# Masks moved into spare contraction rows of an attention kernel's score products

## The chip, the cores and the metric

The kernel runs on one core of one Trainium2 chip. The metric is the device time of the whole program in microseconds; of several executions the median is given. The core has five engines with an instruction queue each: TensorE (PE; its weight loads are listed apart, as PEld), VectorE (DVE), ScalarE (ACT), GpSimd (POOL) and SyncE (SP), which here only issues transfers.

## The reference

Attention comes first, then a product of two linear layers, then a layer of eight experts of which each token takes two. The change touches only attention. There are 4 batches of 8 heads, 576 positions and 64 values a head.

```
scores = (q @ k.T) / sqrt(64)
scores = where(pos_q // 64 >= pos_k // 64, scores, -1e9)
attn = exp(scores - max(scores)); attn = attn / (sum(attn) + 1e-9)
out = attn @ v
x = concat of the heads, 2304 x 512
x = ((x @ w1) * (x @ w2) @ w3) @ w_out
out = sum over the two best experts e of weight * (relu(x @ e_w1[e]) @ e_w2[e])
```

A block of 64 query positions sees its own block of keys and the ones before it.

## The kernel before, in words

Every float32 product is made of rounded parts ("high", in the type fp32r) and what rounding left ("low"), so that three or four products of parts stand for one. The 32 heads go in 16 pairs; `hp` counts the four pairs of a batch, `n` all of them, and `u` is the parity of a pair's buffers. The first batch is written out, the other three are one hardware loop (`batches`). A head's 576 query rows are five tiles of 128, 128, 128, 128 and 64 rows, and tile `i` takes the keys up to its own end: 128, 256, 384, 512 and 576 (the last in two halves of 288). So a pair has ten steps `t`, five for each of its heads.

At each step TensorE makes the scores of tile `t` (`product`), transposes the probabilities of the tile three steps earlier (`turn`), and makes a part of the previous pair's product with v (`values`, in the order of `values_at`). VectorE takes a tile's maximum (L295), and the low part of transposed probabilities (`low`, L250, four steps behind); ScalarE takes the exponentials (L366) and the high part (`high`, L333, three steps behind).

The inputs of the next pair are made ready beside this. SyncE loads q and k, each twice: the 64 values of a head lie on partitions 0 to 63 and again on 64 to 127, both heads side by side, 1152 columns in all. For pair n+1, while pair n is computed:

- GpSimd scales q (L208), once it has cut v of the pair before.
- VectorE rounds q into `q_split` (`q_part`, L273, at step 1) and k into `k_high` (`k_part`, L277, at step 3).
- GpSimd writes what rounding left of q over the upper 64 partitions of `q_split` (L213), and then what is left of k into `k_low` (L217).
- GpSimd then cuts v into its parts (`cut_v`, L226 and L229, two of each).

Since `q_split` holds q's high part on its lower and the low part on its upper 64 contraction rows, and `k_high` holds k twice, one multiplication gives (q_high + q_low) k_high and a second one (q_high + q_low) k_low. Between them stands a third, for tiles 0 to 3: `mask_rows` times `mask_keys`, 64 columns wide, with one contraction row that is not zero, which adds -1e9 to the upper right quarter of the tile's last 128 columns (L399). The fifth tile of keys has 64 positions, and `values` multiplies it over 64 contraction rows (`K = rows[c]`).

At the start, VectorE alone prepares pair 0, once all of its q and k have landed (L307 to L313). The two engines' waits are counted in `q_scaled`, `q_high_ready`, `k_high_ready`, `q_cut` and `k_cut`.

After attention (from about 260 us) come the weights' fusion, the gated product with the routing, and the experts; all of their work starts behind a barrier at attention's end.

Of the kernel before, what the change touches and what calls it, by code (L numbers as in the profile page):

```python
# [5 lines left out]
F32 = mybir.dt.float32  # L6
F32R = mybir.dt.float32r
# [8 lines left out]
def attention(nc, qT, kT, v, identity, xT, prefetch, prefetched):  # L16
# [14 lines left out]
    MASKED = -1e9  # L31
    SCALE = D ** -0.5
    BANKS = 4
# [25 lines left out]
    with ExitStack() as ctx:  # L59
# [9 lines left out]
        q_split = [sb(f"q_split{u}", [P, 2, S], F32R) for u in range(2)]  # L69
        k_high = [sb(f"k_high{u}", [P, 2, S], F32R) for u in range(2)]  # L70
        k_low = [sb(f"k_low{u}", [P, 2, S], F32R) for u in range(2)]
# [6 lines left out]
        mask_rows = sb("mask_rows", [P, P], F32R)  # L78
        mask_keys = sb("mask_keys", [P, BLOCK], F32R)
        mask_raw = sb("mask_raw", [P, P + BLOCK])  # L80
# [16 lines left out]
        waited_pe = sem("waited_pe")  # L97
        qk_loaded = [sem(f"qk_loaded{u}") for u in range(2)]
# [10 lines left out]
        mask_filled = sem("mask_filled")  # L109
        masks_ready = sem("masks_ready")  # L110
        max_found = sem("max_found")
# [9 lines left out]
        out_taken = sem("out_taken")  # L121
        block = ctx.enter_context(nc.Block())
# [14 lines left out]
        def beside(i):  # L137

            return turned[i % TURNED][:, (i + 1) * P:]

# [7 lines left out]
        def _(sp):  # L148
# [11 lines left out]
            for u in range(2):  # L160
                load(u, u)
            sp.dma_start(ident[:], identity).then_inc(ident_loaded, 16)

            def emit(b, first):
                for hp in range(PAIRS):
                    n = b * PAIRS + hp
                    sp.wait_ge(q_cut, n + 1)
                    sp.wait_ge(k_cut, n + 1)

                    load(n + 2, hp % 2)  # L170
                    if first and hp == 0:
                        sp.wait_ge(zeroed, 1)
                    else:
                        sp.wait_ge(v_cut, 2 * n)
# [7 lines left out]
        def _(pool):  # L182
            nc.gpsimd.memset(v_raw[:], 0.0).then_inc(zeroed, 1)
            nc.gpsimd.memset(mask_raw[:], 0.0).then_inc(mask_filled, 1)
            pool.wait_ge(mask_filled, 1)
            nc.gpsimd.memset(mask_raw[0:1, 0:BLOCK], 1.0).then_inc(mask_filled, 1)
            nc.gpsimd.memset(mask_raw[0:1, P:P + BLOCK], MASKED).then_inc(mask_filled, 1)
            nc.gpsimd.memset(scale[:], SCALE).then_inc(zeroed, 1)
            nc.gpsimd.memset(zero[:], 0.0).then_inc(zeroed, 1)
            for u in range(2):  # L190
                nc.gpsimd.memset(row_sum[u][:], 1.0).then_inc(zeroed, 1)
            nc.gpsimd.memset(probs[:], 0.0).then_inc(zeroed, 1)
# [45 lines left out]
            with pool.Fori(1, LAST // 2) as m:  # L238
                for u in range(2):
                    cut_qk(2 * m + u + 1, m + u, 1 - u)  # L240
                    cut_v(2 * m + u, u, False)

        @block.vector
        def _(dve):
# [26 lines left out]
            def q_part(n, u):  # L271
                dve.wait_ge(q_scaled, n + 1)
# [1345 lines left out]
```

## Time and profile before

| | |
|---|---|
| median of three runs | 1150.83 us (1149.87 to 1151.39) |
| the profiled execution: its time | 1149.4 us |
| its span, first to last instruction | 1147.5 us |
| mean granted clock of TensorE | 0.977 |
| busy: PE, PEld, DVE, ACT, POOL | 1078.7, 975.5, 473.9, 371.3, 541.9 us |
| DMA in all | 118.11 MB |

"Busy" is the time in which an engine carries out instructions; a multiplication's end is modelled by the profile, so the start times of neighbours say more of its pace than its duration. In a list in order of time, a row gives start and duration in microseconds, engine, line, operation, the tiles written and read with their shapes (partitions x elements), and in brackets how long the engine had been idle and what it waited for. For a multiplication, 64*128 stands for 64 contraction rows and 128 columns of weights.

### The profile page before, as it was taken

The page shows a single profiled execution, that of the slowest core. Times are in us where ns is not written, and L with a number is a line of the kernel's source. Part 1 is how long each engine was busy: PE and PEld are TensorE (multiplying, and loading weights), DVE is VectorE, ACT ScalarE, POOL GpSimd, SP SyncE. Part 2 cuts the span into 40 slices and gives each one's busy share as a digit, 9 for nine tenths or more (in the row PEclk, how much of TensorE's full clock was granted, in tenths as well). Part 3 has the DMA queues.
Part 4 walks back from the last instruction along what each step waited for, and adds up shares of the span by engine and source line. Part 5 has one row for each costly group of instructions (what it writes and reads, how often), then busy time and mean ns, then how long its engine had stood idle before and what let it go on. Part 6 is the DMA issues. An engine that isn't in the chain of part 4 may idle for free. (4 is left out here: it accounts for less than half of the span.)

```text
span 1147.5 us, 18575 instructions
## 1 busy us (share of the span) xinstructions
PE 1078.7 (94%) x6320; PEld 975.5 (85%) x6321; DVE 473.9 (41%) x1073; ACT 371.3 (32%) x898; POOL 541.9 (47%) x368
## 2 busy tenths in 40 slices
PE   4999999998999999999999549999999999999997
PEld 3888888887798989899999449898989898989895
DVE  5887877866512424241414442222222222222221
ACT  3777777765411213231313142121212121212110
POOL 7776777740000020201111133786878787877752
PEclk9999999998999999999999759999999999999999
DMA  8644444426397010101000063535353535353303
GB/s 230 149 100 92 94 93 101 103 52 195 91 368 278 2 55 0 55 9 46 21 35 34 30 231 128 114 97 144 100 143 117 121 115 123 110 128 119 46 1 46
DMA packets 69638, 118.11 MB, mean 103 GB/s; under 512 B 7776, under 2 KB 25312, under 8 KB 69600
## 3 DMA queue, kind: packets, MB, share of 16 engines
q1 hardware_dynamic: 60960, 97.61, 28.8%
q0 software_dynamic: 8640, 20.00, 8.8%
q8 instruction: 22, 0.36, 0.1%
q14 instruction: 16, 0.13, 0.0%
HBM read 81.00 MB, written 36.59 MB: 102 GB/s over the span
## 5 line engine op out<-in xcount | busy, mean ns | idle before, releaser
L782 POOL DMA_INDIRECT expert_rows<-x_rows,slot_idx x36 | 40.1, 1113 | 311.9 <-DVE slot_idx L925 302.8
L1387 PE MATMUL ps_hT<-xT_high,ew_high 128*128 128x256 f32 (+3 forms) x512 | 156.8, 306 | 1.9 <-DVE xT_low L1473 1.9
L1387 PE MATMUL ps_hT<-xT_low,ew_high 128*128 128x256 f32 (+3 forms) x512 | 155.7, 304 | 0.0
L1387 PE MATMUL ps_hT<-xT_high,ew_low 128*128 128x256 f32 (+3 forms) x512 | 155.2, 303 | 0.0
L1404 PE MATMUL ps_y<-ew_high,hT_high 128*128 128x512 f32 x320 | 129.3, 404 | 1.4 <-DVE hT_low L1480 1.4
L1404 PE MATMUL ps_y<-ew_low,hT_high 128*128 128x512 f32 x320 | 126.9, 397 | 0.0
L1404 PE MATMUL ps_y<-ew_high,hT_low 128*128 128x512 f32 x320 | 126.9, 396 | 0.0
L1480 DVE SCALAR_TENSOR_TENSOR hT_low<-ps_hT,hT_high 128x384 fp32r<-128x384 f32 (+1 forms) x128 | 62.9, 492 | 152.2 <-ACT hT_high L1442 152.2
L1442 ACT ACTIVATE hT_high<-ps_hT 128x384 fp32r<-128x384 f32 (+1 forms) x128 | 56.0, 438 | 156.7 <-PE ps_hT L1387 156.2
L1277 POOL DMA_INDIRECT out<-y_tile,out_rows x40 | 63.1, 1577 | 90.1 <-DVE y_tile L1489 85.8
L1489 DVE TENSOR_SCALAR y_tile<-ps_y,weight_of 128x512 f32<-128x512 f32 x40 | 30.0, 751 | 179.0 <-PE ps_y L1404 179.0
L366 ACT ACTIVATE probs<-scores,neg_max 128x128 f32<-128x128 f32 (+4 forms) x160 | 91.7, 573 | 32.7 <-DVE neg_max L295 32.1
L1387 PEld LDWEIGHTS ps_hT<-xT_high,ew_high 128*128 128x128 f32 x512 | 97.1, 190 | 2.3 <-DVE xT_low L1473 2.3
L1387 PEld LDWEIGHTS ps_hT<-xT_high,ew_low 128*128 128x128 f32 x512 | 97.9, 191 | 0.0
L1387 PEld LDWEIGHTS ps_hT<-xT_low,ew_high 128*128 128x128 f32 x512 | 97.1, 190 | 0.0
L250 DVE TENSOR_TENSOR pT_low<-turned,pT_high 128x128 fp32r<-128x128 f32 (+4 forms) x160 | 76.9, 481 | 29.7 <-ACT pT_high L333 29.7
L1436 ACT CAST xT_high<-ps_xT 128x512 fp32r<-128x512 f32 x40 | 23.5, 587 | 196.4 <-PE ps_xT L1370 196.4
L295 DVE TENSOR_REDUCE neg_max<-scores 128x1 f32<-128x128 f32 (+4 forms) x160 | 85.4, 534 | 3.6 <-PE scores L400 2.4
L932 DVE TENSOR_TENSOR prod<-ps_b,prod 128x384 f32<-128x384 f32 x48 | 26.8, 558 | 130.5 <-ACT prod L811 130.5
L333 ACT CAST pT_high<-turned 128x128 fp32r<-128x128 f32 (+4 forms) x160 | 67.5, 422 | 39.8 <-PE turned L413 35.6
L396 PE MATMUL scores<-k_high,q_split 128*128 128x128 f32 (+2 forms) x192 | 65.7, 347 | 14.1 <-DMA ident_a<-const_in 14.1
L413 PE MATMUL turned<-ident_a,probs 128*128 128x128 f32 (+1 forms) x480 | 73.9, 262 | 4.2 <-DVE pT_low L250 3.2
(198 smaller groups left out, 2683.4 us busy)
## 6 DMA issues: line engine op xcount, KB each, us to landing
spare<-e_w SPq DMA_DIRECT2D x16, 1024.0 KB, 5.3
w_raw<-e_w SPq DMA_DIRECT2D x16, 1024.0 KB, 8.3
q_raw<-qT SPq DMA_DIRECT2D x36, 288.0 KB, 4.3
k_raw<-kT SPq DMA_DIRECT2D x36, 288.0 KB, 5.5
expert_rows<-zeros SPq DMA_DIRECT2D x8, 1290.0 KB, 14.3
ex_rows<-expert_rows SPq DMA_DIRECT2D x40, 258.0 KB, 3.9
out<-zeros SPq DMA_DIRECT2D x11, 512.0 KB, 10.8
v_raw<-v SPq DMA_DIRECT2D x16, 256.0 KB, 4.9
```

Source lines behind the costliest of these rows:

```text
L250: nc.vector.tensor_tensor(pT_low[j][:, 0:i + 1, i * P:i * P + R], turned[t % TURNED][:, 0:(i + 1) * R].rearrange("p (c r) -> p c r", r=R), ...
L295: nc.vector.tensor_reduce(neg_max[0:rows[i], t:t + 1], tile_scores(t), AX.XY if width[i] > 512 else AX.X, ALU.max, negate=True).then_inc(m ...
L333: nc.scalar.copy(pT_high[j][:, 0:i + 1, i * P:i * P + R], turned[t % TURNED][:, 0:(i + 1) * R].rearrange("p (c r) -> p c r", r=R)).then_in ...
L366: nc.scalar.activation(like_scores(probs[0:R, slot, 0:W], t), tile_scores(t), ACT.Exp, bias=neg_max[0:R, t:t + 1], accum_out=row_sum[hp % ...
L396: nc.tensor.matmul(out, lhsT, k_high[u][:, j, a:a + step], start=True, stop=False)
L413: mm = nc.tensor.transpose(turned[t % TURNED][:, c * R:(c + 1) * R], probs[0:R, slot, c * P:(c + 1) * P], ident[0:R, 0:R])
L782: nc.gpsimd.indirect_dma_start(out=rows_dram, out_offset=bass.IndirectOffsetOnAxis(ap=slot_idx[:, k, t:t + 1], axis=0), in_=x_rows[:, t, : ...
L1277: nc.gpsimd.indirect_dma_start(out=out, out_offset=bass.IndirectOffsetOnAxis(ap=out_rows[:, j:j + 1], axis=0), in_=y_tile[j][:], in_offset ...
L1387: mm = nc.tensor.matmul(ps_hT[q % HS][:, 0:rows.stop - rows.start], lhsT[:, c, f * P:(f + 1) * P], rhs[:, c, rows], start=(n == 0), stop=( ...
L1404: mm = nc.tensor.matmul(ps_y[j % YS][:], lhsT[:, f, rows], rhs[:, f], start=(n == 0), stop=(n == 3 * FC - 1))
L1442: nc.scalar.activation(hT_high[:, f, rows], ps_hT[q % HS][:, 0:rows.stop - rows.start], ACT.Relu).then_inc(hhigh, 1)
L1480: nc.vector.scalar_tensor_tensor(out=hT_low[:, f, rows], in0=ps_hT[q % HS][:, 0:rows.stop - rows.start], scalar=0.0, in1=hT_high[:, f, row ...
```

## The change

1. **Masks.** `q_split`, `k_high` and `k_low` are replaced by four tiles. `q_high` holds q's high part on both halves of the partitions. `q_rest` holds q's low part on partitions 0 to 63, and on 64 to 67 four mask rows, loaded from the host once (zeros above). `k_parts` holds k's high part on 0 to 63 and its low part on 64 to 127. `k_again` holds k's high part on 0 to 63 and four mask rows on 64 to 67. So q_high times k_parts gives q_high k_high + q_high k_low, and q_rest times k_again gives q_low k_high and the mask. The masking multiplication is gone, and so is the product of the two low parts.
2. **The copy.** k's high part must stand in `k_again` too. GpSimd issues a DMA from `k_parts` (64 partitions of 4608 bytes) for each pair from 1 on, between its two subtractions; TensorE waits for it (`k_copied`) at step 0. GpSimd's subtraction for k now covers 64 partitions and not 128.
3. **The order of the casts.** k is rounded at step 1 and q at step 2; before, it was q at step 1 and k at step 3.
4. **The fifth key tile** is multiplied over all 128 contraction rows (the upper ones are zero).
5. **The first pair** is loaded head by head, q by SyncE and k by ScalarE's queue, and split head by head by ScalarE and VectorE together. ScalarE also copies the masks into place (four copies of 4 partitions x 1152), after GpSimd has cleared the four tiles.

The diff, cut to its core:

```diff
-        q_split = [sb(f"q_split{u}", [P, 2, S], F32R) for u in range(2)]
-        k_high = [sb(f"k_high{u}", [P, 2, S], F32R) for u in range(2)]
-        k_low = [sb(f"k_low{u}", [P, 2, S], F32R) for u in range(2)]
+        q_high = [sb(f"q_high{u}", [P, 2, S], F32R) for u in range(2)]
+        q_rest = [sb(f"q_rest{u}", [P, 2, S], F32R) for u in range(2)]
+        k_parts = [sb(f"k_parts{u}", [P, 2, S], F32R) for u in range(2)]
+        k_again = [sb(f"k_again{u}", [P, 2, S], F32R) for u in range(2)]
...
-        mask_rows = sb("mask_rows", [P, P], F32R)
-        mask_keys = sb("mask_keys", [P, BLOCK], F32R)
-        mask_raw = sb("mask_raw", [P, P + BLOCK])
...
+        mask_raw = [xT[D:D + MASKS, side, 0:2 * S].rearrange("p (h s) -> p h s", h=2) for side in range(2)]
...
+        def load_first(engine, dst, src, h):
+
+            for half in range(2):
+                engine.dma_start(dst[half * D:(half + 1) * D, h], src[0, h]).then_inc(first_loaded[h], 16)
...
-            for u in range(2):
-                load(u, u)
-            sp.dma_start(ident[:], identity).then_inc(ident_loaded, 16)
+            for side in range(2):
+                sp.dma_start(mask_raw[side], masks[side]).then_inc(masks_loaded, 16)
+            for h in range(2):
+                load_first(sp, q_raw[0], qT, h)
+                if h == 0:
+                    sp.dma_start(ident[:], identity).then_inc(ident_loaded, 16)
+            load(1, 1)
...
-                    sp.wait_ge(q_cut, n + 1)
-                    sp.wait_ge(k_cut, n + 1)
+                    if first and hp == 0:
+                        sp.wait_ge(first_cut, 4)
+                        sp.wait_ge(first_k_again, 2)
+                    else:
+                        sp.wait_ge(q_cut, n)
+                        sp.wait_ge(k_cut, n)
...
-                        sp.wait_ge(zeroed, 1)
+                        sp.wait_ge(zeroed, 4)
...
         def _(pool):
+            nc.gpsimd.memset(q_rest[0][:].bitcast(F32), 0.0).then_inc(masks_zeroed, 1)
+            nc.gpsimd.memset(k_again[0][:].bitcast(F32), 0.0).then_inc(masks_zeroed, 1)
+            nc.gpsimd.memset(q_rest[1][:].bitcast(F32), 0.0).then_inc(masks_zeroed, 1)
+            nc.gpsimd.memset(k_again[1][:].bitcast(F32), 0.0).then_inc(masks_zeroed, 1)
+            nc.gpsimd.memset(probs[:, PSLOTS - 1, S:TILES * P], 0.0).then_inc(zeroed, 1)
+            for u in range(2):
+                nc.gpsimd.memset(row_sum[u][:], 1.0).then_inc(zeroed, 1)
             nc.gpsimd.memset(v_raw[:], 0.0).then_inc(zeroed, 1)
-            nc.gpsimd.memset(mask_raw[:], 0.0).then_inc(mask_filled, 1)
-            pool.wait_ge(mask_filled, 1)
-            nc.gpsimd.memset(mask_raw[0:1, 0:BLOCK], 1.0).then_inc(mask_filled, 1)
-            nc.gpsimd.memset(mask_raw[0:1, P:P + BLOCK], MASKED).then_inc(mask_filled, 1)
             nc.gpsimd.memset(scale[:], SCALE).then_inc(zeroed, 1)
             nc.gpsimd.memset(zero[:], 0.0).then_inc(zeroed, 1)
-            for u in range(2):
-                nc.gpsimd.memset(row_sum[u][:], 1.0).then_inc(zeroed, 1)
-            nc.gpsimd.memset(probs[:], 0.0).then_inc(zeroed, 1)
             for u in range(2):
                 nc.gpsimd.memset(v_high[u][:].bitcast(F32), 0.0).then_inc(zeroed, 1)
             for u in range(2):
                 nc.gpsimd.memset(v_low[u][:].bitcast(F32), 0.0).then_inc(zeroed, 1)
 
...
-                pool.wait_ge(qk_loaded[u], 64 * (half + 1))
+                pool.wait_ge(qk_loaded[u], 64 * (half + u))
                 if first:
-                    pool.wait_ge(zeroed, 9)
-                    pool.wait_ge(q_high_ready, 1)
+                    pool.wait_ge(zeroed, 10)
+                    pool.wait_ge(masks_zeroed, 4)
...
-                if first:
-                    pool.wait_ge(k_cut, 1)
-                    pool.wait_ge(q_cut, 1)
-                pool.wait_ge(q_high_ready, n + 1)
-                nc.gpsimd.tensor_tensor(q_split[u][D:2 * D], q_raw[u][D:2 * D], q_split[u][D:2 * D].bitcast(F32),
-                                        ALU.subtract).then_inc(q_cut, 1)
-                pool.wait_ge(k_high_ready, n + 1)
-                pool.wait_ge(q_cut, n + 1)
-                nc.gpsimd.tensor_tensor(k_low[u][:], k_raw[u][:], k_high[u][:].bitcast(F32), ALU.subtract).then_inc(k_cut, 1)
+                pool.wait_ge(q_high_ready, n)
+                nc.gpsimd.tensor_tensor(q_rest[u][0:D], q_raw[u][0:D], q_high[u][0:D].bitcast(F32), ALU.subtract).then_inc(q_cut, 1)
+                pool.wait_ge(k_high_ready, n)
+                pool.sem_inc(waited_pool, 1)
+                nc.gpsimd.dma_start(k_again[u][0:D], k_parts[u][0:D]).then_inc(k_copied, 16)
+                nc.gpsimd.tensor_tensor(k_parts[u][D:2 * D], k_raw[u][D:2 * D], k_parts[u][D:2 * D].bitcast(F32),
+                                        ALU.subtract).then_inc(k_cut, 1)
...
-                pool.wait_ge(k_cut, n + 2)
...
+            pool.wait_ge(k_copied, 16 * LAST)
...
-                dve.wait_ge(q_scaled, n + 1)
-                nc.vector.tensor_copy(q_split[u][:], q_raw[u][:]).then_inc(q_high_ready, 1)
+                dve.wait_ge(q_scaled, n)
+                nc.vector.tensor_copy(q_high[u][:], q_raw[u][:]).then_inc(q_high_ready, 1)
...
-                dve.wait_ge(qk_loaded[u], 64 * (half + 1))
-                nc.vector.tensor_copy(k_high[u][:], k_raw[u][:]).then_inc(k_high_ready, 1)
+                dve.wait_ge(qk_loaded[u], 64 * (half + u))
+                nc.vector.tensor_copy(k_parts[u][:], k_raw[u][:]).then_inc(k_high_ready, 1)
...
                         if t == 1:
+                            k_part(b * (PAIRS // 2) + (hp + 1) // 2, (hp + 1) % 2)
+                        if t == 2:
                             q_part(n + 1, (hp + 1) % 2)
-                        if t == 3:
-                            k_part(b * (PAIRS // 2) + (hp + 1) // 2, (hp + 1) % 2)
-
-
-            dve.wait_ge(qk_loaded[0], 64)
-            nc.vector.tensor_scalar(q_raw[0][:], q_raw[0][:], SCALE, None, ALU.mult).then_inc(q_scaled, 1)
-            k_part(0, 0)
-            q_part(0, 0)
-            dve.wait_ge(k_high_ready, 1)
-            nc.vector.tensor_tensor(k_low[0][:], k_raw[0][:], k_high[0][:].bitcast(F32), ALU.subtract).then_inc(k_cut, 1)
-            dve.wait_ge(q_high_ready, 1)
-            nc.vector.tensor_tensor(q_split[0][D:2 * D], q_raw[0][D:2 * D], q_split[0][D:2 * D].bitcast(F32),
-                                    ALU.subtract).then_inc(q_cut, 1)
+
+
+            dve.wait_ge(masks_zeroed, 1)
+            for h in range(2):
+                dve.wait_ge(first_loaded[h], 64)
+                nc.vector.tensor_scalar(q_high[0][:, h], q_raw[0][:, h], SCALE, None, ALU.mult).then_inc(first_q_high, 1)
+                dve.wait_ge(first_k_high, h + 1)
+                nc.vector.tensor_tensor(k_parts[0][D:2 * D, h], k_raw[0][D:2 * D, h], k_parts[0][D:2 * D, h].bitcast(F32), ALU.subtract)\
+                    .then_inc(first_cut, 1)
+                dve.wait_ge(first_q_high, h + 1)
+                nc.vector.scalar_tensor_tensor(out=q_rest[0][0:D, h], in0=q_raw[0][0:D, h], scalar=SCALE,
+                                               in1=q_high[0][0:D, h].bitcast(F32), op0=ALU.mult, op1=ALU.subtract).then_inc(first_cut, 1)
...
+                            act.wait_ge(zeroed, 3)
...
-            act.wait_ge(mask_filled, 3)
-            nc.scalar.copy(mask_rows[:], mask_raw[:, 0:P]).then_inc(masks_ready, 1)
-            nc.scalar.copy(mask_keys[:], mask_raw[:, P:P + BLOCK]).then_inc(masks_ready, 1)
+            load_first(act, k_raw[0], kT, 0)
+            load_first(act, k_raw[0], kT, 1)
+            act.wait_ge(masks_loaded, 32)
+            for u in range(2):
+                act.wait_ge(masks_zeroed, 2 * u + 2)
+                nc.scalar.copy(q_rest[u][D:D + MASKS], mask_raw[0]).then_inc(masks_ready, 1)
+                nc.scalar.copy(k_again[u][D:D + MASKS], mask_raw[1]).then_inc(masks_ready, 1)
+            for h in range(2):
+                act.wait_ge(first_loaded[h], 64)
+                nc.scalar.copy(k_parts[0][:, h], k_raw[0][:, h]).then_inc(first_k_high, 1)
+                nc.scalar.copy(k_again[0][0:D, h], k_raw[0][0:D, h]).then_inc(first_k_again, 1)
...
-                if t == 0:
-                    pe.wait_ge(k_cut, n + 1)
-                    pe.wait_ge(q_cut, n + 1)
+                if fresh and i == 0:
+                    pe.wait_ge(first_cut, 2 * j + 2)
+                    pe.wait_ge(first_k_again, j + 1)
+                elif t == 0:
+                    pe.wait_ge(k_cut, n)
+                    pe.wait_ge(q_cut, n)
+                    pe.wait_ge(k_copied, 16 * n)
...
-                lhsT = q_split[u][:, j, i * P:i * P + R]
+                rows_of = slice(i * P, i * P + R)
                 step = HALF if W > 512 else W
                 for a in range(0, W, step):
                     out = scores[0:R, bank[t] + a // step, 0:step]
-                    nc.tensor.matmul(out, lhsT, k_high[u][:, j, a:a + step], start=True, stop=False)
-                    if i < FULL:
-
-                        nc.tensor.matmul(scores[0:R, bank[t], W - BLOCK:W], mask_rows[:], mask_keys[:], start=False, stop=False)
-                    mm = nc.tensor.matmul(out, lhsT, k_low[u][:, j, a:a + step], start=False, stop=True)
+                    nc.tensor.matmul(out, q_high[u][:, j, rows_of], k_parts[u][:, j, a:a + step], start=True, stop=False)
+                    mm = nc.tensor.matmul(out, q_rest[u][:, j, rows_of], k_again[u][:, j, a:a + step], start=False, stop=True)
...
-                K = rows[c]
...
-                    lhsT, rhs = vs[u][0:K, c, j], ps[j][0:K, c]
+                    lhsT, rhs = vs[u][:, c, j], ps[j][:, c]
...
-            pe.wait_ge(masks_ready, 2)
+            pe.wait_ge(masks_ready, 4)
...
+    block = 64
+    place = np.arange(S)
+    masks = np.zeros((2, S // (2 * block), 2, S), np.float32)
+    for i in range(S // (2 * block)):
+        masks[0, i, :, place // block == 2 * i] = 1
+        masks[1, i, :, place // block == 2 * i + 1] = -1e9
```

## Rows read from the trace of the kernel before

**Rows 1.** The page: busy time in tenths of 40 equal slices, TensorE's row.
```profile
PE   4999999998999999999999549999999999999997
```
**Rows 2.** Busy time by engine in a stretch of attention (instructions in brackets), granted clock, DMA share, GB/s.
```profile
180.00:210.00 30.00, 29.89 (x209) 26.74 (x208) 24.04 (x54) 21.91 (x67) 21.42 (x15) 1.00 0.45 98
```
**Rows 3.** Waits from 60 to 240 us: total, times, longest.
```profile
POOL q_split L213 <- DVE q_split L273: 40.7, 13, 3.6
```
**Rows 4.** GpSimd in order of time, one pair: start, duration, instruction, wait before it.
```profile
104.60 2.64 POOL L213 TENSOR_TENSOR q_split<-q_raw,q_split 64x1152 fp32r<-64x1152 f32 x1 [3.59 <-DVE q_split L273]
107.94 2.65 POOL L217 TENSOR_TENSOR k_low<-k_raw,k_high 128x1152 fp32r<-128x1152 f32 x1 [0.70 <-DVE k_high L277]
110.81 0.72 POOL L226 TENSOR_TENSOR v_high<-v_raw,zero_a 128x320 fp32r<-128x320 f32 x1 [0.23 <-POOL k_low L217]
112.56 0.72 POOL L226 TENSOR_TENSOR v_high<-v_raw,zero_a 128x320 fp32r<-128x320 f32 x1
114.29 2.11 POOL L208 TENSOR_TENSOR q_raw<-q_raw,scale 128x1152 f32<-128x1152 f32 x1
119.54 2.65 POOL L213 TENSOR_TENSOR q_split<-q_raw,q_split 64x1152 fp32r<-64x1152 f32 x1 [3.14 <-DVE q_split L273]
```
**Rows 5.** VectorE in order of time, around both casts of the same pair.
```profile
103.77 0.75 DVE L273 CAST q_split<-q_raw 128x1152 fp32r<-128x1152 f32 x1
104.43 0.69 DVE L250 TENSOR_TENSOR pT_low<-turned,pT_high 128x512 fp32r<-128x512 f32 x1
105.03 0.55 DVE L295 TENSOR_REDUCE neg_max<-scores 128x1 f32<-128x384 f32 x1
105.50 0.48 DVE L250 TENSOR_TENSOR pT_low<-turned,pT_high 128x320 fp32r<-128x320 f32 x1
106.77 1.09 DVE L277 CAST k_high<-k_raw 128x1152 fp32r<-128x1152 f32 x1
107.78 0.28 DVE L250 TENSOR_TENSOR pT_low<-turned,pT_high 128x128 fp32r<-128x128 f32 x1
```
**Rows 6.** TensorE's multiplications in order of time, same pair.
```profile
106.49 0.27 PE L447 MATMUL heads_out<-pT_high,v_low 128*128 128x192 f32 x1
106.61 0.27 PE L447 MATMUL heads_out<-pT_low,v_high 128*128 128x192 f32 x1
106.81 0.29 PE L447 MATMUL heads_out<-pT_high,v_high 64*128 64x64 f32 x1
...
110.15 0.28 PE L396 MATMUL scores<-k_high,q_split 128*128 128x256 f32 x1
110.27 0.19 PE L399 MATMUL scores<-mask_keys,mask_rows 128*128 128x64 f32 x1
...
110.49 0.60 PE L413 MATMUL turned<-ident_a,probs 128*128 128x128 f32 x4
...
115.40 0.30 PE L396 MATMUL scores<-k_high,q_split 128*128 128x128 f32 x1
```
**Rows 7.** GpSimd in order of time, in the expert stage.
```profile
714.93 4.61 POOL L1239 TENSOR_TENSOR ew_low<-spare,ew_high 128x2048 fp32r<-128x2048 f32 x1
719.71 1.69 POOL L1277 DMA_INDIRECT out<-y_tile,out_rows  x1 [0.16 <-issue]
720.87 4.16 POOL L1233 TENSOR_TENSOR ew_high<-spare,consts 128x2048 fp32r<-128x2048 f32 x1
...
752.40 3.60 POOL L1233 TENSOR_TENSOR ew_high<-w_raw,consts 128x2048 fp32r<-128x2048 f32 x1
```
**Rows 8.** Instructions of one tensor (ns: min/median/max), and its DMAs' time to landing.
```profile
L782 POOL DMA_INDIRECT expert_rows<-x_rows,slot_idx x36: 963/969/2225, 403.3 to 663.4; - x36
...
DMA to landing us min/median/max: 2.6/3.0/17.1
```
**Rows 9.** All engines in order of time, at the start.
```profile
13.96 2.10 POOL L208 TENSOR_TENSOR q_raw<-q_raw,scale 128x1152 f32<-128x1152 f32 x1 [4.90 <-DMA k_raw<-kT]
14.11 0.48 PE L396 MATMUL scores<-k_high,q_split 128*128 128x128 f32 x1 [14.11 <-DMA ident_a<-const_in]
...
17.18 2.64 POOL L213 TENSOR_TENSOR q_split<-q_raw,q_split 64x1152 fp32r<-64x1152 f32 x1 [1.12 <-DVE q_split L273]
...
18.32 2.12 DVE L277 CAST k_high<-k_raw 128x1152 fp32r<-128x1152 f32 x1
```
**Rows 10.** VectorE in order of time, in the last pair.
```profile
239.55 0.48 DVE L250 TENSOR_TENSOR pT_low<-turned,pT_high 128x320 fp32r<-128x320 f32 x1
```

More of the change, by code:

```diff
@@ L13, with attention @@
 META = 4
-def attention(nc, qT, kT, v, identity, xT, prefetch, prefetched):
+def attention(nc, qT, kT, v, identity, masks, xT, prefetch, prefetched):
     _, _, D, S = qT.shape
@@ L30, in attention @@
     HALF = S // 2
-    MASKED = -1e9
     SCALE = D ** -0.5
+    MASKS = masks.shape[1]
     BANKS = 4
@@ L97, in attention @@
         waited_pe = sem("waited_pe")
+        waited_pool = sem("waited_pool")
         qk_loaded = [sem(f"qk_loaded{u}") for u in range(2)]
@@ L108, in attention @@
         scores_ready = sem("scores_ready")
-        mask_filled = sem("mask_filled")
+        masks_loaded = sem("masks_loaded")
+        masks_zeroed = sem("masks_zeroed")
         masks_ready = sem("masks_ready")
+        first_loaded = [sem(f"first_loaded{h}") for h in range(2)]
+        first_k_high = sem("first_k_high")
+        first_k_again = sem("first_k_again")
+        first_q_high = sem("first_q_high")
+        first_cut = sem("first_cut")
+        k_copied = sem("k_copied")
         max_found = sem("max_found")
@@ L208, in cut_qk @@
                 nc.gpsimd.tensor_tensor(flat, flat, scale[:].to_broadcast([P, 2 * S]), ALU.mult).then_inc(q_scaled, 1)
-                if first:
-                    pool.wait_ge(k_cut, 1)
-                    pool.wait_ge(q_cut, 1)
-                pool.wait_ge(q_high_ready, n + 1)
-                nc.gpsimd.tensor_tensor(q_split[u][D:2 * D], q_raw[u][D:2 * D], q_split[u][D:2 * D].bitcast(F32),
-                                        ALU.subtract).then_inc(q_cut, 1)
-                pool.wait_ge(k_high_ready, n + 1)
-                pool.wait_ge(q_cut, n + 1)
-                nc.gpsimd.tensor_tensor(k_low[u][:], k_raw[u][:], k_high[u][:].bitcast(F32), ALU.subtract).then_inc(k_cut, 1)
+                pool.wait_ge(q_high_ready, n)
[5 more added lines that the diff above has]
+                                        ALU.subtract).then_inc(k_cut, 1)
             def cut_v(n, u, first):
                 pool.wait_ge(v_loaded, 32 * (n + 1))
-                pool.wait_ge(k_cut, n + 2)
+                pool.wait_ge(k_cut, n + 1)
                 if not first:
@@ L364, in emit @@
                         elif t == 0:
-                            act.wait_ge(zeroed, 6)
+                            act.wait_ge(zeroed, 3)
                         nc.scalar.activation(like_scores(probs[0:R, slot, 0:W], t), tile_scores(t), ACT.Exp,
                                              bias=neg_max[0:R, t:t + 1], accum_out=row_sum[hp % 2][0:R, t:t + 1]).then_inc(exp_done, 1)
-            act.wait_ge(mask_filled, 3)
-            nc.scalar.copy(mask_rows[:], mask_raw[:, 0:P]).then_inc(masks_ready, 1)
-            nc.scalar.copy(mask_keys[:], mask_raw[:, P:P + BLOCK]).then_inc(masks_ready, 1)
+            load_first(act, k_raw[0], kT, 0)
[9 more added lines that the diff above has]
+                nc.scalar.copy(k_again[0][0:D, h], k_raw[0][0:D, h]).then_inc(first_k_again, 1)
             batches(act, emit)
@@ L1505, in _, with bass_attention_moe @@
             through(dve, stretch)
-def bass_attention_moe(nc, qT, kT, v, w1, w2, w3T, w_out, w_gate_noise, noise, e_w1, e_w2, const_in, C, out):
+def bass_attention_moe(nc, qT, kT, v, w1, w2, w3T, w_out, w_gate_noise, noise, e_w1, e_w2, const_in, masks, C, out):
     P = 128
@@ L1547, in bass_attention_moe @@
                          (consts[:], const_in), (counts[:], const_in[:, C["start"]:C["start"] + E])]
-            attention(nc, qT, kT, v, const_in[:, C["ident"]:C["ident"] + P], xT, prefetch, prefetched)
+            attention(nc, qT, kT, v, const_in[:, C["ident"]:C["ident"] + P], masks, xT, prefetch, prefetched)
             w1_high, w1_low, w2_high, w2_low = (part(moe, name, DC, F) for name in ("w1_high", "w1_low", "w2_high", "w2_low"))
@@ L1610 @@
         "const_in": const,
+        "masks": masks,
     }
```

## The prediction

> **What bounds the kernel now.** I read the page's slices first: TensorE is busy in nearly every slice up to the last, so a saving in attention shortens the kernel only if it ends attention sooner, and what follows then moves up as a whole, since it starts behind a barrier [rows 1]. The table by stretch says what holds attention: in 30 us TensorE is busy for 29.89, VectorE for 24.04, ScalarE for 21.91 and GpSimd for 21.42 [rows 2]. TensorE is the bound. The waits show where the others have air: GpSimd waits for q's cast 13 times, 40.7 us in all, so 3.1 us a pair, and that is its whole reserve [rows 3]. Last I read one pair in order of time on GpSimd, VectorE and TensorE [rows 4 to 6]. A pair lasts 14.94 us there, from one subtraction for q to the next (104.60 to 119.54) [rows 4].
>
> **Masks and fifth tile: what TensorE saves.** The trace has the price of a masking multiplication in start times. In the tile of 256 keys the first product starts at 110.15 and the transposes that follow all three at 110.49: 0.34 us. The first of them handed over after 0.12, so two without a mask take about 0.24, and the mask costs 0.10 to 0.11. Eight a pair: 0.9 us. In `values` a multiplication of 192 columns hands over after 0.12 (106.49 to 106.61), but the one before the switch to 64 rows after 0.20 (106.61 to 106.81) [rows 6]. I take 0.08 for each change of row count, two a head, four a pair: 0.3 us. So TensorE needs 1.2 us less: 14.9 - 1.2 = 13.7 us a pair. The bounds are 0, if the weight loads hide otherwise, and 0.15 a mask with 0.2 more for a pair's four changes, which gives about 13.2. The product of the low parts that is dropped costs nothing either way: both forms have two full multiplications a tile.
>
> **The casts: a lock seen in the rows.** k's cast is the same instruction as q's in shape, but takes 1.09 us against 0.75. GpSimd's subtraction runs from 104.60 to 107.24; the cast is issued at 106.77 and ends 0.62 after GpSimd does [rows 4, 5]. At the start it is plainer: 2.12 us, from 18.32 to 20.44, which is 0.62 behind GpSimd's end at 19.82 [rows 9]. So a cast of VectorE does not run beside GpSimd's arithmetic; it waits for the instruction's end. The Trainium skill says the same on its page "SBUF — State Buffer", section "SBUF: two separate sides": the port pair of the two engines is an exclusive lock, held for the full instruction. By that rule the trace agrees.
>
> **The new loop.** The moved casts save GpSimd its 0.70 us wait for k, and make VectorE meet the scaling of q instead. Follow one pair from the start C of q's cast. Before, GpSimd's subtraction starts at C + 0.83 (103.77 to 104.60), and from there to the end of the scaling it is 11.80 (104.60 to 116.40), of which 0.70 is the wait for k [rows 4, 5]. After, k is already rounded, but the DMA issue stands between the subtractions. Call what it holds GpSimd up D. Then the scaling ends at E = C + 0.83 + 11.80 - 0.70 + D = C + 11.93 + D; 0.05 less on average, since the gap before L226 shows only in every other pair. Call it 11.88 + D.
>
> VectorE comes to k's cast one low part, one maximum and the cast itself ahead of q's cast. If TensorE set the pace at 13.7, that is at C + 13.7 - 1.7 = C + 12.0. With D over 0.1 the scaling still runs, so the cast waits for E. The next instruction starts 0.53 after E (107.78 behind 107.25), the low part of 512 takes 0.60 to the next start (104.43 to 105.03), the maximum of 384 takes 0.47 (105.03 to 105.50) [rows 4, 5]; then q's cast starts the next round. The period of this ring is 11.88 + D + 0.53 + 0.60 + 0.47 = 13.48 + D. It has no reserve: GpSimd waits for VectorE's q, and VectorE waits for GpSimd's port.
>
> **What D is.** No direct DMA is issued by GpSimd before. The nearest rows are indirect ones of 128 rows. Between two expert instructions one runs 1.69 us; the instruction before ends at 719.54 and the one after at 725.03 where alone it takes 3.60, so it is held up 1.89, the DMA's duration and 0.20 [rows 7]. The other kind takes 0.97 [rows 8]. This one has 64 rows and no index to read. I take two thirds of the 0.97, 0.66, and the 0.20: D = 0.86. Below, the bound is 0 (the descriptors are written beside the next instruction), above it is 1.89. The period is 14.34. The page named above gives 620 ns for such a DMA alone; by that D would be 0.82 and the time 0.6 us less than below.
>
> The copy's landing: issued near C + 3.5, landing 3.0 later in the median of the indirect DMAs [rows 8], while TensorE's step 0 comes some 11.6 us after C (103.77 to 115.40) [rows 5, 6]. It is hidden by 5 us. GpSimd's cut of v ends 2.1 before E, near C + 10.6, and is wanted at about the same step 0: hidden by one. SyncE's loads wait for the same cuts as before and have a pair's time.
>
> **The start.** Pair 0 is ready sooner; TensorE now begins at 14.11 [rows 9]. But pair 1 lands at 13.96, the bytes ahead of it are the same, and GpSimd's scaling takes 2.10: until 16.06 VectorE cannot cast beside it. Then 0.53 and the maximum's 0.47 (pair 0 has no low part at step 2): the first C is 17.1. The head-by-head load thus wins almost nothing that lasts; it ends in the wait for pair 1. What covers the four mask copies is the same wait.
>
> **The sum.** The last of 16 casts of q starts at 17.1 + 15 x 14.34 = 232.2, and VectorE goes on after 0.67, at 232.9. The same place before, the low part behind the maximum of step 2 in the last pair, is at 239.55 [rows 10]: 6.7 us sooner. From there on no ring binds; five masks (0.5) and the changes of three heads (0.5) are saved: 1.0. In all 7.7 us. The span goes from 1147.5 to 1139.8, the profiled execution from 1149.4 to 1141.7, and the median of 1150.83, which stands 1.4 over the profiled one, to 1143.1.
>
> **Rivals.** A measurement of this kernel tells about 0.2% from no change, 2.3 us.
>
> *A, the forecast:* the ring binds with D from 0.5 to 1.2. By the same sum 1137.7 to 1148.2. Chance 0.48.
>
> *B, TensorE stays the bound:* D does not hold GpSimd up (under 0.5), or the cast slips in before the scaling. At 13.7 a pair the last cast is at 222.6, 16.3 sooner, and with the 1.0 it is 1133.5; with the upper bound of the mask's price the ring without D, 13.48, gives 1130. For it: GpSimd's next instruction is shown starting 1.16 after the DMA's start, while the DMA lasts 1.69; against it: that instruction is longer by the difference [rows 7]. Chance 0.29.
>
> *C, no change:* D between 1.22 and 1.52. The ring then lasts what a pair lasts now; the sum breaks even at 14.85, D = 1.37. Chance 0.12.
>
> *D, slower:* the same ring with D over 1.52. At 1.89 it lasts 15.37, the last cast is at 247.7, and the kernel takes 1158.6. It decides by this one price: is a direct DMA of 64 rows as dear as the dearest indirect one of 128? Against it: the cheap kind is half of that. A copy that lands too late for step 0 would be shown by TensorE's wait; it needs 8 us, more than twice the median. Chance 0.11.
>
> Faster 0.77, same 0.12, slower 0.11. The range that leaves out two in ten, nearly all of it above and at the far end of B: 1131 to 1151. The forecast's own range is 1137.7 to 1148.2.
>
> **What the profile would show.** Right: GpSimd's subtractions 3.5 us apart; k's cast longer than 0.75, ending 0.6 behind the scaling; GpSimd idle for 2.4 us before its subtraction for q (1.60 of VectorE's work and 0.83); periods of 14.3; TensorE idle for 0.5 us or more a pair; no 64*128 products with v. B would show k's cast at 0.75, periods of 13.7, and TensorE without idle time. The prediction is wrong in its ground if the cast of k doesn't wait for the scaling although it runs, wrong in size if D is not 0.86, and wrong at the start if pair 1 lands elsewhere than at 14.

## The result, and the profile after

The changed kernel takes 1153.74 us, the median of 7 runs (1151.66 to 1154.91), beside 1150.91 us for the kernel before on the same chip (7 runs). The ratio is 1.0024, with a 95% interval of 1.0013 to 1.0035: slower by 0.24%, where 1143.1 us was forecast. The profiled span is 1150.0 us (1147.5 before).

The same stretch of attention, in the table by stretch of the kernel after:

```profile
180.00:210.00 30.00, 27.66 (x190) 23.70 (x190) 25.70 (x52) 21.05 (x67) 21.73 (x17) 1.00 0.53 114
```

TensorE is busy for 27.66 of the 30 us where it was 29.89 [rows 2]. It is no longer the bound; it stands idle for 1.2 us a pair. VectorE is busy for 25.70 where it was 24.04, although it does the same instructions. The waits from 60 to 240 us (total, times, longest):

```profile
POOL q_rest L229 <- DVE q_high L291: 41.6, 12, 3.6
ACT probs L385 <- DVE neg_max L313: 37.5, 45, 2.0
PE heads_out L472 <- POOL v_low L246: 8.1, 11, 0.8
DVE row_den L275 <- ACT probs L385: 4.0, 11, 0.4
```

GpSimd's wait for q's cast is 3.5 us a pair; it was 3.1 [rows 3], and 2.4 was forecast. The third row was not forecast at all: TensorE waits for v's low part once in nearly every pair.

GpSimd in order of time, one pair:

```profile
94.53 2.65 POOL L229 TENSOR_TENSOR q_rest<-q_raw,q_high 64x1152 fp32r<-64x1152 f32 x1 [3.56 <-DVE q_high L291]
97.14 0.56 POOL L232 DMA_DIRECT2D k_again<-k_parts  x1
97.77 2.66 POOL L233 TENSOR_TENSOR k_parts<-k_raw,k_parts 64x1152 fp32r<-64x1152 f32 x1
...
104.05 2.11 POOL L227 TENSOR_TENSOR q_raw<-q_raw,scale 128x1152 f32<-128x1152 f32 x1
109.72 2.65 POOL L229 TENSOR_TENSOR q_rest<-q_raw,q_high 64x1152 fp32r<-64x1152 f32 x1 [3.56 <-DVE q_high L291]
```

And VectorE in the same pair:

```profile
93.71 0.74 DVE L291 CAST q_high<-q_raw 128x1152 fp32r<-128x1152 f32 x1
...
104.34 1.85 DVE L275 TENSOR_SCALAR row_den<-row_sum 128x10 f32<-128x10 f32 x1 [0.37 <-ACT probs L385]
106.10 0.28 DVE L313 TENSOR_REDUCE neg_max<-scores 128x1 f32<-128x128 f32 x1
...
107.17 0.74 DVE L295 CAST k_parts<-k_raw 128x1152 fp32r<-128x1152 f32 x1
107.83 0.68 DVE L268 TENSOR_TENSOR pT_low<-turned,pT_high 128x512 fp32r<-128x512 f32 x1
...
108.90 0.74 DVE L291 CAST q_high<-q_raw 128x1152 fp32r<-128x1152 f32 x1
```

There is a ring of the two engines, as forecast. GpSimd works from 94.53, 0.82 behind the start of q's cast (93.71), to the end of the scaling (104.05 + 2.11 = 106.16) without a gap worth naming; VectorE is held until that very moment, and from there it needs until 108.90 for the next cast of q. But it is not k's cast that is held. That one comes at 107.17, when GpSimd has been done for a microsecond, and takes 0.74 us. Held is `row_den`, the addition of 1e-9 to 10 row sums per partition: 1.85 us for an instruction of 128 x 10 elements, which ends at 106.19, 0.03 behind the scaling. It stands at step 0, so VectorE still has 2.74 us of work between the end of the scaling and q's cast, and not the 1.60 of the forecast. From the start of the DMA's issue to the next instruction are 0.63 us (97.14 to 97.77), less than the 0.86 assumed. So the ring is 12.45 (93.71 to 106.16) and 2.74: 15.19. The mean of the last twelve pairs, from one subtraction for q to the next, is 15.23, where the kernel before has 14.91.

The start, VectorE, GpSimd and TensorE in order of time, and the table by stretch behind the second pair's begin:

```profile
13.57 0.74 DVE L295 CAST k_parts<-k_raw 128x1152 fp32r<-128x1152 f32 x1
```

```profile
13.52 2.75 POOL L227 TENSOR_TENSOR q_raw<-q_raw,scale 128x1152 f32<-128x1152 f32 x1 [3.26 <-DMA k_raw<-kT]
...
19.71 0.75 POOL L232 DMA_DIRECT2D k_again<-k_parts  x1
```

```profile
11.43 0.45 PE L427 MATMUL scores<-k_parts,q_high 128*128 128x128 f32 x1 [11.43 <-ACT k_again L398]
...
27.27 0.45 PE L427 MATMUL scores<-k_parts,q_high 128*128 128x128 f32 x1 [3.51 <-DMA k_again<-k_parts]
```

```profile
28.00:32.00 4.00, 4.00 (x17) 3.83 (x16) 2.80 (x6) 1.26 (x4) 0.96 (x1) 0.50 1.06 328
```

TensorE begins 2.7 us sooner (14.11 before [rows 9]). But the first copy of k is issued at 19.71, when SyncE has issued most of the loads for the next stage, and TensorE goes on only at 27.27, after 3.51 us without work. Behind that pause the granted clock is 0.50, its lower level of 1.2 GHz; it is 0.50 from 20 to 23 us too, behind a pause of 1.73 us that ends at 18.01, and 1.00 again from 34 us. The kernel before has 1.00 from 14 to 40 us. The first period lasts 17.58 us.

Attention's last instruction on `xT` ends at 264.7 instead of 260.1, 4.6 later. The experts' first product starts 4.3 later, their last ends 2.6 later.

### The profile page after: what moved, and what is told of

Same layout as the page of the kernel before. It is cut to its first block and busy times, and to the rows that moved or that the text cites. A ratio compares the mean times of both kernels' runs of the same rounds, so it can differ in the third digit from the quotient of the medians.

```text
span 1150.0 us, 18346 instructions
## 1 busy us (share of the span) xinstructions
PE 1064.3 (93%) x6192; PEld 954.7 (83%) x6193; DVE 485.0 (42%) x1074; ACT 376.4 (33%) x904; POOL 552.1 (48%) x385
## 5 line engine op out<-in xcount | busy, mean ns | idle before, releaser
L441 PE MATMUL turned<-ident_a,probs 128*128 128x128 f32 (+1 forms) x480 | 75.0, 265 | 10.6 <-DVE pT_low L268 7.9
L427 PE MATMUL scores<-k_parts,q_high 128*128 128x128 f32 (+2 forms) x192 | 66.1, 349 | 14.9 <-ACT k_again L398 11.4
L838 ACT COPY prod<-ps_a 128x384 f32<-128x384 f32 x48 | 23.0, 479 | 167.1 <-PE ps_b L1034 167.1
```

Of the source, the lines that this page charges most:

```text
L427: nc.tensor.matmul(out, q_high[u][:, j, rows_of], k_parts[u][:, j, a:a + step], start=True, stop=False)
L441: mm = nc.tensor.transpose(turned[t % TURNED][:, c * R:(c + 1) * R], probs[0:R, slot, c * P:(c + 1) * P], ident[0:R, 0:R])
```

## The experiments

Ratios are to the kernel before, on the same chip, with 95% intervals. "Period" is the mean of the last twelve pairs; it is 14.91 us before and 15.23 after. In the diffs, "..." stands for lines left out.

**1. The row-sum addition left out.** The reciprocal reads the sum itself. The sums are at least 1, so that 1e-9 changes no bit.

```diff
-nc.vector.tensor_scalar(row_den[:], row_sum[hp % 2][:], 1e-9, None, ALU.add).then_inc(den_ready, 1)
...
-nc.vector.reciprocal(row_inv[:], row_den[:]).then_inc(inv_ready, 1)
+nc.vector.reciprocal(row_inv[:], row_sum[hp % 2][:]).then_inc(inv_ready, 1)
```

> The changed kernel without the addition of 1e-9 to the row sums (a sum is at least 1, so the addition changes no bit of it); the reciprocal reads the sums directly. Theory T1: the pair of 15.2 us is a ring of GpSimd and VectorE, closed where this small addition at step 0 waits for GpSimd's scaling of q to end. Without it the next instruction that needs the port is k's cast at step 1, 1.14 us of VectorE's work later, so the period should fall from 15.2 to 14.05 and the time by about 15 x 1.1 = 17 us, to some 1137 (0.988 of before). If the reciprocal takes the port too, it will show 1.5 us or more in the addition's place and the gain is about 0.2 us a pair. Rival T2: TensorE's wait for v's low part (0.8 us a pair) holds the pair; then the period stays at 15.2 and the time at 1153.

Measured: 0.9903 [0.9887, 0.9919], 1140.24 us; period 14.12. One instruction of 10 elements a partition is worth 1.1 us a pair. Only VectorE's work was changed, so TensorE's wait for v's low part, 0.8 us a pair in the kernel after, did not set the 15.23. VectorE and GpSimd at one such place, and a row of the waits from 60 to 240 us:

```profile
129.79 0.22 DVE L274 RECIPROCAL row_inv<-row_sum 128x10 f32<-128x10 f32 x1
...
130.96 0.75 DVE L290 CAST k_parts<-k_raw 128x1152 fp32r<-128x1152 f32 x1
...
132.69 0.75 DVE L286 CAST q_high<-q_raw 128x1152 fp32r<-128x1152 f32 x1
```

```profile
128.88 2.11 POOL L227 TENSOR_TENSOR q_raw<-q_raw,scale 128x1152 f32<-128x1152 f32 x1
```

```profile
PEld heads_out L464 <- POOL v_low L246: 4.6, 12, 0.5
```

The reciprocal runs in 0.22 us in the middle of the scaling (128.88 to 130.99). It isn't held; the addition of the same size is. k's cast comes at 130.96, just as the scaling ends, and q's cast 1.70 behind that end. But this is not yet the forecast's ring shown at work: k's cast takes 0.75 us here and 0.80 to 0.83 in every other pair, so it is held by 0.08 at most, while the weight load for v's product waits for GpSimd's cut of v in each pair. A ring of nearly the same length runs through that product; run 7 shows it.

**2. No copy of k.** The DMA and the waits for it are gone; `k_again` keeps what it held, so the product with q's low part has old keys.

```diff
-nc.gpsimd.dma_start(k_again[u][0:D], k_parts[u][0:D]).then_inc(k_copied, 16)
...
-pe.wait_ge(k_copied, 16 * n)
```

> The changed kernel without the DMA that copies k's high part into the second tile, and without TensorE's wait for it (the product of q's low part is then with old or zero keys). T1: the DMA is one link of the ring, 0.63 us from start to start of its neighbours; the period falls to 14.6 and the time by 15 x 0.63 = 9.5 us, to 1144 (0.994). The row sum's addition still ends just behind the scaling. T2: v's cut comes 0.63 sooner as well, so the same gain; this run tells the two only from a third, that the DMA's traffic or its landing holds TensorE, in which case the gain would differ from 0.63 a pair.

Measured: 0.9960 [0.9946, 0.9974], 1146.87 us; period 14.73, first period 14.78. The ring gives back 0.50 a pair, and not 0.63: without the DMA GpSimd's subtraction for k starts 2.73 us behind the one for q (106.19 to 108.92), with it 3.24 (94.53 to 97.77), so the DMA holds GpSimd up by 0.51. `row_den` is still held, and lasts 1.3 to 1.5 us.

**3. The casts where they were**, all else as after: q at step 1, k at step 3.

```diff
 if t == 1:
-    k_part(...)
-if t == 2:
     q_part(...)
+if t == 3:
+    k_part(...)
```

> The changed kernel with q rounded at step 1 and k at step 3, as before the change. T1: in the ring, q's cast comes 1.73 us sooner behind the scaling (1.01 in place of 2.74), while GpSimd waits 0.7 for k again between its subtractions. Period 15.19 - 1.73 + 0.70 = 14.16, time about 15 us less than the changed kernel: 1138 (0.989). T2: v's cut ends 0.7 later behind q's cast but starts one step sooner; a gain of about 1 us a pair too. A third theory, that the moved casts are harmless and the copy alone costs, would give 1153 or more.

Measured: 0.9966 [0.9955, 0.9978], 1147.82 us; period 14.77, where 14.16 was expected. GpSimd and VectorE:

```profile
121.30 2.65 POOL L229 TENSOR_TENSOR q_rest<-q_raw,q_high 64x1152 fp32r<-64x1152 f32 x1 [1.83 <-DVE q_high L291]
125.16 0.56 POOL L232 DMA_DIRECT2D k_again<-k_parts  x1 [1.21 <-DVE k_parts L295]
```

```profile
118.44 1.06 DVE L275 TENSOR_SCALAR row_den<-row_sum 128x10 f32<-128x10 f32 x1 [0.37 <-ACT probs L385]
...
120.48 0.74 DVE L291 CAST q_high<-q_raw 128x1152 fp32r<-128x1152 f32 x1
...
123.20 1.37 DVE L295 CAST k_parts<-k_raw 128x1152 fp32r<-128x1152 f32 x1
```

The addition is still held by the scaling, and k's cast now by the subtraction. GpSimd's wait ahead of the DMA is 1.21, where the one ahead of an arithmetic instruction was 0.70 [rows 4]. That half microsecond is most of the miss of 0.61. With everything else changed, moving the casts thus costs 0.46 us a pair.

**4. The fifth tile over 128 rows, alone in the kernel before.**

```diff
-K = rows[c]
...
-lhsT, rhs = vs[u][0:K, c, j], ps[j][0:K, c]
+lhsT, rhs = vs[u][:, c, j], ps[j][:, c]
```

> The kernel before with only the fifth key tile multiplied over 128 rows. TensorE is the bound there; each of four changes of row count a pair should give back 0.08 to 0.09 us: 0.33 us a pair, 5 us in all, 1145.6 (0.9955). If the row count is free on TensorE, no change.

Measured: 0.9926 [0.9911, 0.9941], 1143.55 us; period 14.44. The part saves 0.47 us a pair, half as much again as forecast.

**5. The masking multiplications left out of the kernel before** (the output is unmasked).

```diff
-if i < FULL:
-    nc.tensor.matmul(scores[0:R, bank[t], W - BLOCK:W], mask_rows[:], mask_keys[:], start=False, stop=False)
```

> The kernel before with the masking multiplication left out (so every query sees its whole last tile). It gives the price of the 128 masking multiplications where TensorE is the bound: by the rows of before 0.10 to 0.11 us each, 8 a pair, 0.9 us a pair; period 14.91 to about 14.0, time about 13.5 us less, 1137.5 (0.988). If the lock of the two engines binds first, GpSimd will show a row sum's addition of a microsecond or more and the period stays above 14.2.

Measured: 0.9912 [0.9896, 0.9929], 1141.01 us; period 14.22, 0.69 less, where 0.9 was expected.

**6. The loads for the next stage behind pair 1's v, all else as after.**

```diff
-if first and hp == 0:
+if first and hp == 1:
```

> The changed kernel with one line changed: SyncE issues the five loads for the next stage behind pair 1's v instead of pair 0's. Theory: the first copy of k's high part, issued at 19.7 us, queues behind these 3 MB, lands at 27.3, and TensorE stands for 3.5 us and then runs for some 6 us at the lower clock. Moved, that copy should land in about 3 us, and the first period falls from 17.6 to the ring's 15.2: 2.4 us less than the changed kernel, 1151.3 (0.9995 to 1.000). If the first period is long for another reason, nothing changes.

Measured: 1.0029 [1.0017, 1.0042], 1153.50 us, no better than the changed kernel, where 2.4 us less was expected. The first period falls from 17.58 to 15.33, but the second is 17.78: the loads only meet the next copy, which lands after 8.7 us. DMA issues to `k_again`, from issue to landing:

```profile
DMA to landing us min/median/max: 3.1/3.1/8.7
```

**7. As 1 and 6, and q scaled by ScalarE** at step 7 (for the second pair at step 1 of the first), so that GpSimd has no scaling.

```diff
+nc.scalar.activation(q_raw[u][:], q_raw[u][:], ACT.Copy, scale=SCALE).then_inc(q_scaled, 1)
...
-nc.gpsimd.tensor_tensor(flat, flat, scale[:].to_broadcast([P, 2 * S]), ALU.mult).then_inc(q_scaled, 1)
```

> The changed kernel with three edits: the addition of 1e-9 to the row sums is left out (it changes no bit), the loads for the next stage go behind pair 1's v, and q is scaled by ScalarE (once a pair, at step 7) and not by GpSimd. T1: GpSimd then has 10.3 us of work a pair and no link to VectorE's small instructions; the ring is open, and TensorE is the bound again at 13.3 to 13.6 a pair. Attention ends about 20 us sooner than before: 1131 (0.983). If ScalarE's extra 1.1 us a pair tells, the period is 13.7 to 14.

Measured: 0.9907 [0.9889, 0.9926], 1140.12 us; period 14.13, where 13.3 to 13.6 was expected; run 1 has 14.12. The first ring is gone, and a second one shows, on VectorE, GpSimd and TensorE, and in the waits from 60 to 240 us:

```profile
119.54 0.75 DVE L281 CAST q_high<-q_raw 128x1152 fp32r<-128x1152 f32 x1
...
133.54 0.75 DVE L281 CAST q_high<-q_raw 128x1152 fp32r<-128x1152 f32 x1
```

```profile
129.01 0.87 POOL L241 TENSOR_TENSOR v_low<-v_raw,v_high 128x320 fp32r<-128x320 f32 x1
```

```profile
129.94 0.33 PE L468 MATMUL heads_out<-pT_high,v_high 128*128 128x128 f32 x1 [0.32 <-POOL v_low L241]
```

```profile
PEld heads_out L468 <- POOL v_low L241: 4.7, 12, 0.7
```

From q's cast at 119.54 GpSimd's cut of v ends at 129.88, 10.34 later; TensorE's multiplication with v waits for it, and q's cast follows 3.66 behind: 14.00. In the next pair the product starts just behind the cut again (143.93 behind 143.87), and q's cast follows 3.95 behind it: 14.28. The two kinds alternate. With q rounded at step 2 the cut of v is late for step 0. Since this kernel has no scaling on GpSimd and the same period as run 1, the second ring alone is enough for 14.13.

**8. As 1 and 3 together:** no addition, casts at steps 1 and 3.

> The changed kernel without the addition to the row sums, and with q rounded at step 1 and k at step 3. T1: q's cast then starts right behind the scaling (0.1 in place of 1.60), and GpSimd waits 1.21 before the copy (measured with the old order), so the ring takes 0.82 + 2.65 + 1.21 + 0.63 + 2.79 + 3.49 + 2.11 + 0.1 = 13.8; TensorE's own time is about 13.5. Period 13.8 to 13.9 against 14.12 with the new order; the time 3 to 4 us less than the 1140.2 of the run without the addition alone, 1136.5.

Measured: 0.9857 [0.9835, 0.9878], 1134.63 us; period 13.89. As expected, and 1.4% faster than the kernel before.

**9. As 8, and the loads for the next stage spread** over two pairs, one behind pair 1's v and four behind pair 2's.

> The changed kernel without the addition to the row sums, with q rounded at step 1 and k at step 3, and with the five loads for the next stage spread: the 2 MB of w_out behind pair 1's v, the other four behind pair 2's. Moved as a block to pair 1 they only made pair 2's copy late in place of pair 1's (8.7 us to landing, second period 17.8). Spread, no copy should take over 4 us to land and no period should be above 14.5, so 2 to 4 us less than the same kernel with the loads behind pair 0: near 1131.5 (0.984). If the w_out load alone still collides, one period of about 16 stays.

Measured: 0.9856 [0.9838, 0.9873], 1133.76 us; period 13.90. The first period is 14.03 instead of 15.88, and in the profile attention ends 2.1 us sooner than in 8, but the two ratios can't be told apart. One copy still takes 5.9 us to land, where 4 at most was expected.

**10. Fifth tile and no masks in the kernel before:** edits 4 and 5 together.

> The kernel before with the fifth key tile over 128 rows and the masking multiplication left out: TensorE's program is then that of the changed kernel, with neither the copy nor the new order of the casts. One alone gave 0.47 and the other 0.71 us a pair. If TensorE is the only bound, both give 1.18: period 13.73, time about 20 us less, 1131 (0.982). If the chain of maximum, exponential, transposition and parts, or the lock, has come up to it, the period stays at 13.9 to 14.1 and the time at 1135 to 1137.

Measured: 0.9879 [0.9860, 0.9898], 1138.29 us; period 13.98. Alone they save 0.47 and 0.69, together 0.93.

**11. Control: the row-sum addition left out of the kernel before.**

> The kernel before without the addition of 1e-9 to the row sums. There the addition never met GpSimd (0.17 us each, but for the second pair's 1.55), and TensorE is the bound: no change, 0.999 to 1.001. If the addition costs by itself and not through the lock, 15 us less as in the changed kernel.

Measured: 0.9987 [0.9976, 0.9999], 1149.13 us; period 14.86. Where TensorE is the bound the addition costs next to nothing.

**12. As 9, and q scaled by ScalarE.**

> As the first kernel of this batch, and q scaled by ScalarE at step 7. With the casts at steps 1 and 2 this stayed at 14.13 a pair though GpSimd waited 4.6 us: a second ring, q's cast, GpSimd's cuts, v's low part 10.35 later, TensorE's wait for it at step 0 and the 3.66 from there to the cast at step 2, 14.0. With q's cast at step 1 that ring is 11.6 + 1.9 = 13.5, so TensorE's own 13.7 should hold: 1 to 3 us less than the first kernel of this batch. If ScalarE's 1.15 us a pair lies in the chain, it is the same or slower.

Measured: 0.9853 [0.9836, 0.9870], 1133.61 us; period 13.91. No different from 9, although GpSimd is busy for only 18.27 us in the stretch from 180 to 210 us:

```profile
180.00:210.00 30.00, 29.10 (x207) 25.76 (x206) 25.68 (x56) 26.11 (x77) 18.27 (x15) 1.00 0.62 136
```

TensorE is busy for 29.10 of 30 us here. Versions 8, 9, 10 and 12 all end between 13.89 and 13.98.

## Why the prediction was wrong

**The step that failed** is "VectorE comes to k's cast one low part, one maximum and the cast itself ahead of q's cast" and what hangs on it, VectorE's 1.60 us in the ring. The ring has no reserve, as forecast, but it closes at the first instruction of VectorE that is held after GpSimd has begun to scale, and that is the row-sum addition at step 0. VectorE's share is 2.74, 1.14 more. Shown by run 1: without the addition the period falls by 1.11 and the share is 1.70. The kernel before gave the sign, in its second pair; VectorE, then GpSimd:

```profile
27.44 1.55 DVE L257 TENSOR_SCALAR row_den<-row_sum 128x10 f32<-128x10 f32 x1 [0.37 <-ACT probs L366]
```

```profile
26.86 2.11 POOL L208 TENSOR_TENSOR q_raw<-q_raw,scale 128x1152 f32<-128x1152 f32 x1
```

An instruction of 10 elements a partition lasts 1.55 us and ends 0.02 behind the scaling. It is the only one of 16 so long; the others take 0.17. The prediction counted only the casts among the instructions that take the lock. The Trainium skill, in its page "SBUF — State Buffer", section "Who interferes with whom", lists tensor_scalar beside copy and cast as operations that can take the shared pair. The trace agrees, with 1.85 us here.

**D**, on which all the chances hung, was 0.63 from issue to next start, and 0.51 by run 2, not 0.86. GpSimd's whole part, from q's cast to the end of the scaling, was 12.45 where 12.74 was forecast, 0.29 shorter. So 14.34 - 0.29 + 1.14 = 15.19. The kernel came out slower, as in rival D, but not by its cause: D was below the forecast's, and the length was VectorE's. With the measured 12.45 and the forecast's own 1.60 the ring would have been 14.05, an estimate; run 1, at 14.12, comes near it, but there the second ring is as long.

**The start** was wrong twice. The first cast of q came at 16.31, 0.8 sooner than forecast. The forecast had VectorE wait for the first scaling; instead k's cast, issued 0.05 behind it, ran its 0.74 us at once, and the scaling took 2.75 in place of 2.11. Runs 1, 2 and 6 show the same (2.67 to 2.95). By the prediction's own words a cast of k that doesn't wait for the scaling speaks against its ground; but the scaling grew by 0.64 us, nearly the cast's length, so it looks as if only the order was the other one and GpSimd was held. And the copy's landing, which "needs 8 us, more than twice the median" to be late, took 7.3 for the first pair, since some 3 MB of loads had been issued in the 3 us before it. The forecast took the median of 3.0 and passed over the longest landing in the same row, 17.1 [rows 8]. The first period was 17.58, 3.24 more than the forecast's. Run 2 (no copy, first period 14.78, so 2.80 of the 3.24), run 6 (the loads moved, the collision moved with them) and run 9 (spread, 14.03) show it.

**The sum, redone.** VectorE was to go on at 232.9 in the last pair and does so at 246.64. The start gives -0.8, the first period +3.24, the 14 others (15.15 on average, 14.34 forecast) +11.3: together the 13.7 of the difference. From there to attention's end 2.5 us are saved, not 1.0; in the kernel before k's cast still comes behind this place (240.74, 1.19 us), which may be part of it, but no run shows that. So attention ends 4.6 later instead of 7.7 sooner. Of the 4.6 only 2.6 are left at the end of the experts and 2.8 in the medians; from the experts' first product to their last is 1.7 us shorter than in the profile before (456.3 against 458.0), where the change has no part. In run 11, whose expert code is that of before, it is 457.2. What makes these differences stays open.

**v's cut "hidden by one"** was wrong by nearly two: TensorE waits 0.7 to 0.8 us for it in nearly every pair. The cut ended 10.3 us behind the start of q's cast, 10.6 forecast; but the forecast had step 0 come 11.6 behind it, a distance read in the kernel before, where q is rounded at step 1 and not at step 2. In the kernel after TensorE is ready for v 9.5 to 9.6 behind. Run 7 shows that this would have held the pairs at 14.0 and 14.28 in turn anyway, so that with q's cast at step 2 rival B's 13.7 was out of reach.

**What TensorE saves.** The fifth tile was 0.47 for 0.3, the masks 0.69 for 0.9, together 0.93 for 1.2. In start times of the kernel after, the change of row count is gone: of the last two products with v the first hands over after 0.11 (0.20 before [rows 6]).

```profile
109.35 0.27 PE L474 MATMUL heads_out<-pT_low,v_high 128*128 128x192 f32 x1
109.46 0.22 PE L474 MATMUL heads_out<-pT_high,v_high 128*128 128x64 f32 x1
```

Why the two savings don't add, and what keeps four different versions at 13.9 to 14.0, was not settled; in run 12 ScalarE took over GpSimd's scaling without a change of the period, so it is not the length of either's work alone.

**What was right:** the lock between VectorE and GpSimd's arithmetic, a ring of the two that takes TensorE's place as the bound, GpSimd's part of it ("E = C + 11.88 + D" gives 12.51 with the measured 0.63, and it was 12.45), and that the head-by-head load wins little.

## What to carry to other kernels

When a cast is moved next to another engine's work, go through every instruction of the moved engine in the window of the lock, not only the large ones, and look in the trace of before for one whose duration varies: 0.17 us here and 1.55 us there is a wait, whatever its size. A copy by DMA that lands in 3.1 us in the median took 7.3 right behind bulk loads here, so the first one must be priced by itself and not by the median. Where a cast is moved, every distance read from it in the old kernel moves too. A saving on the engine that bounds a loop is worth only what lies down to the next chain, and the best version here came from taking one needless instruction off that chain and leaving the casts where they were.

## What the runs showed of the hardware

- TENSOR_SCALAR of 128x10 f32, from SBUF to SBUF, waits for the end of GpSimd's arithmetic (1.85 us, after); RECIPROCAL of a tile of the same size doesn't (0.22 us in the midst of it, run 1).
- The holding goes both ways: where a cast of VectorE starts within 0.3 us of GpSimd's scaling, the cast takes its 0.74 us and the scaling 2.67 to 2.95 in place of 2.11 (the first scaling, in the kernel after and in runs 1, 2 and 6).
- A DMA issue of GpSimd with 64 partitions of 4608 bytes lasts 0.56 us and holds it up by 0.51 (run 2). It lands 3.1 us later in the median, and 7.3 (after) to 8.7 (run 6) behind bulk loads of the same time.
- Behind a wait for VectorE's cast, GpSimd's DMA issue starts 0.5 us later than an arithmetic instruction does: 0.59 us behind the cast's end (run 3) and 0.08 (before). A semaphore increment of GpSimd stands ahead of the issue, and no run tells its part.
- The change between 128 and 64 contraction rows costs TensorE about 0.1 us each time: 0.08 by start times [rows 6], 0.12 by run 4 (0.47 for four).
